# Turned keys and queries with two heads side by side, score products of 64 rows a head, and the low part of x and one mask on other engines

## The chip, the cores and the metric

One core of a Trainium2 chip runs the whole program. The metric is the device time of one execution in microseconds (us), the median of the runs. Engines are named as in the profile: PE is TensorE (matrix products and transposes), PEld its weight loads, DVE VectorE, ACT ScalarE, POOL GpSimd, SP the engine that issues most DMAs.

## The reference

Attention that keeps the 32 largest scores of each row, followed by a gated product, all in float32:

```python
# q, k, v: (4, 8, 576, 64); w_a, w_b: (512, 1536); w_out: (1536, 512)
scores = scale * np.matmul(q, k.transpose(0, 1, 3, 2))
kth = np.partition(scores, -32, axis=-1)[..., -32:-31]
scores = np.where(scores >= kth, scores, -1000000000.0)
scores = scores - np.max(scores, axis=-1, keepdims=True)
attn = np.exp(scores)
attn = attn / (np.sum(attn, axis=-1, keepdims=True) + 1e-09)
x = np.matmul(attn, v).transpose(0, 2, 1, 3).reshape(2304, 512)
out = ((x @ w_a) * (x @ w_b)) @ w_out
```

## The kernel before

**Precision.** A float32 number is split into a high part, which is the number copied to the type fp32r, and a low part, the number minus the high part. Products of fp32r run in one pass over the array. A full product is then three: high by high, high by low, low by high (line 606 for x by w_a and w_b, line 638 for the hidden values by w_out).

**Units and slots.** A unit is 128 queries of a pair of heads (two heads of one batch), or, for the last 64 queries of a batch (the tail), 64 queries of two pairs. There are 72 units: in each of 4 batches 4 blocks of queries by 4 pairs, and 2 tail units. Each engine runs its own program of slots s = 0 to 78, written out by hand, and in slot s it works on different units: DVE finds the 32 largest of unit s, PE makes the scores of unit s+1 (`qk`), turns the probabilities of unit s-1 (`transposes`) and multiplies those of unit s-2 by v (`probs_v`), and the gated product runs 5 slots behind in 72 chunks of 384 columns (chunk n in slot n+5), 4 chunks for each group of 128 tokens. The order inside a slot is fixed; an engine that waits holds up everything behind it.

**PE in slot s:** `probs_v(s-2)`, half of `columns_of(n, 0)` (6 products of 384 columns), `x_subtract(s-2)`, `qk(s+1, 0)`, a part of the keys if one is due (`k_transposes`), the other half of `columns_of(n, 0)`, `qk(s+1, 1)`, `turn_hidden(n-1)`, `transposes(s-1)`, `q_transposes(s+3)`, `output(n-2)` (9 products of 512), `columns_of(n, 1)` (12 products of 384).

**Scores.** A head has 64 rows. The kernel before turns the keys of one head with their high and low part side by side, so that one column of `k_t` holds the high part in rows 0 to 63 and the low part in rows 64 to 127; the query is turned twice over in the same way, and its columns in `q_t` are used with zeros beside them. One product of 128 rows then gives q by (high + low of k); a second, with the low part of q, the rest. Eight products of 288 columns make a unit's scores (16 for a tail unit), in two halves that share the PSUM banks 0 and 1. ACT and POOL split the keys before they are turned (`split_k`, lines 697 and 895), PE turns them in 9 pieces for a pair of heads (line 488), and ACT copies them out (line 709). A pair's keys come in two parts in two slots; there are 12 pairs after the first batch.

**Top 32.** DVE takes the 8 largest four times (line 999) and takes them out in between (line 1016), for both heads of a unit. Then `below` (line 1031) writes `keep` for each head, 0 or -3e38, POOL adds it to the scores (`masked`, line 920), ACT takes the exponential (line 740) and the sum, DVE the inverse (line 1026), and ACT multiplies (line 755). DVE waits for the sums in the middle of the next unit.

**Low part of x.** ACT copies `ps_x` to `x_hi` (line 775), PE subtracts `x_hi` from `ps_x` by a product with the negative identity (line 577), and ACT copies the rest to `x_lo`.

Three score buffers (`ROWS = 3`) let DVE run ahead of PE.

Of the kernel before, what the change touches and what calls it, by code (L numbers as in the profile page):

```python
# [6 lines left out]
def topk_attention_gated_product(nc, q, k, v, w_parts, xs, out):  # L7
    fp32, fp32r = mybir.dt.float32, mybir.dt.float32r
    ALU, ACT = mybir.AluOpType, mybir.ActivationFunctionType

    P = 128
# [16 lines left out]

    PAIR = 2 * S
    TAILS = FULL  # L30

    PARTS_OF_ROW = [(0, FULL * P), (FULL * P, PAIR)]
    KEY_PARTS = [(0, NB * P), (NB * P, PAIR)]
# [47 lines left out]
    NPREPS = 2 * KB * BATCHES  # L81
    PREP_SLOT = [-1] * 4 + [0, 0, 1, 1]
    for b in range(1, BATCHES):
        at = first_unit(b, 0)
        PREP_SLOT += [at + n for n in ((-7, -6, -5, -4, -3, -2, -1, -1) if b % 2 else (-7, -6, -5, -4, -3, -2, -1, 0))]
    for n in range(2 * KB, NPREPS):
        b, p, before = n // 2 // KB, n // 2 % KB, n // 2 - KPAIRS
        assert PREP_SLOT[n] <= first_unit(b, p) - 2
        assert before < 0 or PREP_SLOT[n] >= last_unit(before // KB, before % KB) - 1

# [3 lines left out]
    def split_early(n):  # L94

        return n >= 2 * KB and PREP_SLOT[n - 2] <= PREP_SLOT[n] - 2

    def frees_late(n):

        before = n // 2 - KPAIRS  # L100
        return before >= 0 and PREP_SLOT[n] == last_unit(before // KB, before % KB) - 1

    def parts_until(s):

        return sum(PREP_SLOT[n] <= s for n in range(NPREPS))

# [43 lines left out]
    with ExitStack() as ctx:  # L150
# [13 lines left out]
        neg_ident = sb("neg_ident", [P, P], fp32r)  # L164
        k_rows = [sb("k_rows_a", [P, NB, 2, D]), sb("k_rows_b", [P, FULL, 2, D])]
        q_rows = sb("q_rows", [P, QBUF, 4, 2, D])
        k_t = sb("k_t", [P, KPAIRS, PAIR], fp32r)
        q_t = sb("q_t", [P, 2, 2, 7 * D], fp32r)
        q_whole = sb("q_whole", [P, 2, P])
# [5 lines left out]
        neg_max = sb("neg_max", [P, 2, 2])  # L175
# [3 lines left out]
        probs_t = sb("probs_t", [P, PAIR])  # L179
        x_hi = sb("x_hi", [P, 2, KB, G], fp32r)  # L180
# [6 lines left out]
        leaving = k_t[:, KPAIRS - 1, 0:LOWS * WC].rearrange("p (n c) -> p n c", n=LOWS)  # L187

        ps = ctx.enter_context(nc.psum_tensor("ps", [P, 8, 512], fp32))
        ps_s = ps[:, 0:2, 0:HALF]  # L190
# [6 lines left out]
        ps_q = ps[:, 0:2, HALF:HALF + P]  # L197
# [5 lines left out]
        def keys_in_psum(n):  # L203
            if n < 4:
                return [ps_45, ps_67, ps_67, ps_t][n]
            return ps[:, 6, :] if n == preps_at(PREP_SLOT[n])[0] + 1 else ps_t


        ps_first = [ps[:, 2:4, 0:HALF], ps[:, 4:6, 0:HALF]]
# [3 lines left out]
        def q_columns(u, part):  # L213

            if is_tail(u):
                return q_t[:, u % 2, part, 0:6 * D].rearrange("p (h i c) -> p i h c", h=2, c=D)[:, 0:3:2, :, :]
            return q_t[:, u % 2, part, D:7 * D].rearrange("p (h b c) -> p h b c", h=2, c=D)[:, :, 1:3, :]


        def wo_low(n):  # L220
            if n not in LATE_WO:
                return wo_lo[:]
            at = LATE_WO.index(n) * HB * WC
            return k_t[:].rearrange("p k c -> p (k c)")[:, at:at + HB * WC].rearrange("p (b c) -> p b c", b=HB)
# [13 lines left out]
        def low_of_h(n):  # L238
# [3 lines left out]
            return k_t[:].rearrange("p k c -> p (k c)")[:, at:at + HC]  # L242
# [7 lines left out]
        s_negid = sem("s_negid")  # L250
        ld_k = [sem("ld_ka"), sem("ld_kb")]
# [10 lines left out]
        w_lo_done = sem("w_lo_done")  # L262
        khi_ready = sem("khi_ready")
        klo_ready = sem("klo_ready")
        kt_done = sem("kt_done")
        kt_ready = sem("kt_ready")
# [8 lines left out]
        shift_ready = sem("shift_ready")  # L275
# [11 lines left out]
        xsub_done = sem("xsub_done")  # L287
# [25 lines left out]
        def preps_before(u):  # L313
            b, t, pairs, place = UNITS[u]
            return 2 * (b * KB + max(pairs)) + 2
# [18 lines left out]
        def _(sp):  # L334
            def load_k(n):
                if n >= NPREPS:
                    return
                part = n % 2
                wait(sp, kt_done, n - 1)
                b, p = n // 2 // KB, n // 2 % KB  # L340
                head = b * HEADS + 2 * p
                sp.dma_start(k_rows[part][:, 0:FULL, 1, :],
                             k[head + part, 0:FULL * P, :].rearrange("(t p) d -> p t d", p=P)
                             ).then_inc(ld_k[part], 16)
                if part == 0:
                    for h in range(2):
                        sp.dma_start(k_rows[0][h * TAIL:(h + 1) * TAIL, TAILS, 1, :], k[head + h, FULL * P:S, :]
                                     ).then_inc(ld_k[0], 16)

            def load_q(u):  # L350
# [5 lines left out]
                for twin in range(2):  # L356
                    sp.dma_start(q_rows[0:w, u % QBUF, 0:heads, twin, :],
                                 q[head:head + heads, t * P:t * P + w, :].rearrange("h p d -> p h d")
                                 ).then_inc(ld_q[u % QBUF], 16)

            def load_v(b, p):
# [3 lines left out]
                for h in range(2):  # L365
                    sp.dma_start(v_rows[:, p, 0:FULL, h * D:(h + 1) * D],
                                 v[head + h, 0:FULL * P, :].rearrange("(t p) d -> p t d", p=P)
# [78 lines left out]
            for s in range(FIRST, MOE_END):  # L446
                mine = preps_at(s)
                n = s - MOE0
                for m in range(2, 5):
                    weights(s - 1, m)  # L450
# [630 lines left out]
```

## Time and profile before

| what | us |
|---|---|
| median of 3 runs | 844.06 (843.84 to 845.9) |
| the profiled execution: its time | 845.23 |
| the profiled execution: its span, first to last instruction | 843.4 |
| mean granted TensorE clock | 0.982 of full |

| engine | busy us | share of the span |
|---|---|---|
| PE | 802.1 | 95% |
| PEld | 733.6 | 87% |
| DVE | 772.5 | 92% |
| ACT | 654.2 | 78% |
| POOL | 494.1 | 59% |

Busy time is the union of the instructions' spans; a matmul's span has its latency in it, so a pace is read from starts, or from the chain of work that ended last, which cuts each instruction at the start of the next one.

### The profile page before, as it was taken

What the parts mean: (1) busy time and instruction counts of PE and PEld (TensorE: products, weight loads), DVE (VectorE), ACT (ScalarE), POOL (GpSimd) and SP (SyncE); (2) the same over time, 40 slices, a digit from 0 to 9 for tenths busy, and PEclk for the clock granted to TensorE, in tenths of its full rate; (3) what the DMA queues carried; (4) which work ended last, traced back from release to release, by engine and by line L of the source; (5) the groups of instructions that cost most, each with busy time, mean ns of one, the idle gap of its engine ahead of it and who ended that gap; (6) DMA issues with size and microseconds to landing.
All of it is one profiled execution on the core that took longest, in us unless ns stands there. A gap on an engine that the chain in (4) does not pass through costs nothing.

```text
span 843.4 us, 18267 instructions
## 1 busy us (share of the span) xinstructions
PE 802.1 (95%) x5856; PEld 733.6 (87%) x5856; DVE 772.5 (92%) x1664; ACT 654.2 (78%) x1560; POOL 494.1 (59%) x503
## 2 busy tenths in 40 slices
PE   6458899999999999999999999999999999999998
PEld 4447789989999999999999999998999999999987
DVE  7999999998899999999999999998899999999700
ACT  5888988877778788888877878886777878887632
POOL 3889976655455556566555556665455555555422
PEclk9768999999999999999999999999999999999999
DMA  5576764443554444454644444445363444453562
GB/s 132 151 219 205 228 199 141 118 141 127 153 170 123 146 124 146 124 146 139 166 145 140 130 142 130 135 132 149 110 181 125 141 130 142 126 141 121 149 224 83
DMA packets 136957, 123.88 MB, mean 147 GB/s; under 512 B 81568, under 2 KB 100000, under 8 KB 136864
## 3 DMA queue, kind: packets, MB, share of 16 engines
q1 hardware_dynamic: 136320, 122.58, 49.0%
q8 instruction: 49, 0.80, 0.4%
q14 instruction: 44, 0.36, 0.2%
q10 hardware_dynamic: 544, 0.13, 0.1%
HBM read 113.25 MB, written 9.44 MB: 145 GB/s over the span
## 4 chain that ended last, share of the span: by engine, by line
PE 86%; DVE 7%; SPq 2%; issue 2%; ACT 1%; POOL 1%; DMA 1%; ACTq 0%; POOLq 0%
PE ps L606 35%; PE ps L638 18%; PE ps L566 9%; PE ps L522 9%; PE ps L548 8%; DVE work L1016 3%; PE ps L617 3%; DVE best L999 3%; PE ps L488 2%; PE ps L500 2%; DVE keep L1031 1%; SPq L369 1%; DMA k_rows_a<-in_k 1%; PE ps L577 0%; DMA stage<-in_w 0%
## 5 line engine op out<-in xcount | busy, mean ns | idle before, releaser
L999 DVE MAX8 best<-work 128x8 f32<-128x576 f32 x432 | 305.6, 751 | 0.0
L920 POOL TENSOR_TENSOR scores<-scores,keep 128x576 f32<-128x576 f32 x144 | 218.0, 1534 | 137.1 <-DVE keep L1031 137.1
L1016 DVE MATCH_REPLACE8 work<-best,work 128x576 f32<-128x576 f32 x288 | 213.7, 747 | 0.0
L606 PE MATMUL ps<-w_hi,x_hi 128*128 128x384 f32 x576 | 205.2, 356 | 6.5 <-issue 3.3
L606 PE MATMUL ps<-w_hi,x_lo 128*128 128x384 f32 x576 | 194.7, 338 | 0.0
L927 POOL TENSOR_TENSOR ab<-ab 128x384 f32<-128x384 f32 x72 | 73.3, 1018 | 155.0 <-ACT ab L787 155.0
L606 PE MATMUL ps<-w_lo,x_hi 128*128 128x384 f32 x432 | 146.2, 338 | 0.0
L728 ACT COPY scores<-ps 128x576 f32<-128x576 f32 x142 | 90.8, 640 | 48.6 <-PE ps L522 48.4
L606 PEld LDWEIGHTS ps<-w_hi,x_hi 128*128 128x128 f32 x576 | 108.2, 188 | 22.1 <-issue 15.1
L740 ACT ACTIVATE scores<-scores,neg_max 128x576 f32<-128x576 f32 x144 | 114.2, 808 | 12.6 <-POOL scores L920 12.0
L522 PE MATMUL ps<-k_t,q_t 128*128 128x288 f32 x632 | 116.3, 312 | 4.8 <-ACT scores L728 2.6
L999 DVE MAX8 best<-scores 128x8 f32<-128x576 f32 x144 | 102.3, 753 | 14.0 <-ACT scores L728 11.2
L755 ACT ACTIVATE scores<-scores,inverse 128x576 f32<-128x576 f32 x144 | 112.7, 783 | 2.7 <-DVE inverse L1026 2.4
L606 PEld LDWEIGHTS ps<-w_hi,x_lo 128*128 128x128 f32 x576 | 108.4, 188 | 0.0
L1016 DVE MATCH_REPLACE8 work<-best,scores 128x576 f32<-128x576 f32 x144 | 106.1, 746 | 0.0
L522 PEld LDWEIGHTS ps<-k_t,q_t 128*128 128x128 f32 x632 | 96.7, 197 | 6.9 <-ACT scores L728 4.0
L566 PE MATMUL ps<-probs_t,v_rows 128*64 128x128 f32 (+1 forms) x1600 | 95.1, 267 | 4.2 <-ACT probs_t L765 4.2
L566 PEld LDWEIGHTS ps<-probs_t,v_rows 128*64 128x64 f32 x1600 | 78.5, 137 | 22.4 <-issue 17.0
L638 PE MATMUL ps<-w_hi,h_hi 128*128 128x512 f32 x216 | 91.0, 421 | 0.1
L763 ACT COPY probs_t<-ps 128x512 f32<-128x512 f32 x144 | 81.3, 587 | 10.8 <-PE ps L548 3.4
L548 PE MATMUL ps<-ident,scores 128*128 128x128 f32 x648 | 86.1, 280 | 2.0 <-ACT k_t L709 2.0
L606 PEld LDWEIGHTS ps<-w_lo,x_hi 128*128 128x128 f32 x432 | 81.7, 189 | 3.0
(70 smaller groups left out, 1353.6 us busy)
## 6 DMA issues: line engine op xcount, KB each, us to landing
wo_lo<-x_scratch SPq DMA_DIRECT2D x69, 768.0 KB, 4.5
wb_lo<-x_scratch SPq DMA_DIRECT2D x70, 384.0 KB, 4.1
stage<-in_w SPq DMA_DIRECT2D x36, 256.0 KB, 3.2
q_rows<-in_q SPq DMA_DIRECT2D x142, 64.0 KB, 3.0
x_scratch<-k_t SPq DMA_DIRECT2D x18, 256.0 KB, 2.7
v_rows<-in_v SPq DMA_DIRECT2D x32, 128.0 KB, 2.6
out<-stage SPq DMA_DIRECT2D x16, 256.0 KB, 4.7
k_t<-x_scratch SPq DMA_DIRECT2D x3, 768.0 KB, 6.7
```

The costliest lines, as they stand in the source:

```text
L522: last = mm(ps_s[:, j, :], weights, k_t[:, (b * KB + p) % KPAIRS, at:at + HALF], start=(i == 0), stop=(i == len(terms) - 1))
L548: last = tr(to, row_of(u)[:, at:at + P], ident[:])
L566: last = mm(ps_x[h * D:(h + 1) * D, i * w:(i + 1) * w], v_rows[:, p, block, h * D:(h + 1) * D], probs_t[:, at:at + w], start=(i == 0 and c ...
L606: last = mm(ps_ab[which], x[:, g % 2, kb, :], w, start=(kb == 0 and m == 0), stop=(kb == KB - 1 and m == 2))
L638: last = mm(ps_y, x[:, cols], w, start=(f + b == 0 and m == 0), stop=(f + b == NF - 1 and m == 2))
L728: A.copy(scores[:, u % ROWS, :, half * HALF:(half + 1) * HALF], ps_s[:]).then_inc(s_ready, 1)
L740: A.activation(row, row, ACT.Exp, bias=neg_max[:, u % 2, j:j + 1], scale=SCALE, accum_out=sums[:, u % 2, j:j + 1]).then_inc(e_ready, 1)
L755: A.mul(row, row, inverse[:, u % 2, j:j + 1]).then_inc(p_ready, 1)
L763: A.copy(probs_t[:, a:a + FULL * P], ps[:, 2 + j, :]).then_inc(pt_ready, 1)
L920: V.tensor_tensor(row, row, keep[:, j, :], ALU.add).then_inc(mask_done, 1)
L999: ins = V.max(best[:, u % 2, j, 8 * r:8 * r + 8], src)
L1016: V.match_replace(out=work[:, j, :], in_to_replace=best[:, u % 2, j, 8 * r:8 * r + 8], in_values=src, imm_value=NEG).then_inc(chain, 1)
```

## The change

- `q_transposes` and `k_transposes` turn whole rows with both heads side by side: head 0 in rows 0 to 63, head 1 in rows 64 to 127. Queries take one piece for a unit and not two, keys 5 pieces for a pair of heads and not 9, in one slot. The last piece of the keys has 64 rows.
- The split comes after the turning. ACT copies the turned keys out twice (high part, whole), POOL subtracts; the queries likewise, with 128 columns and not 256.
- `qk` makes three products for each head (high by high, high by low, low by high), each with 64 rows: head 0 in rows 0 to 63, head 1 in rows 64 to 127, in turn. A unit has 12 products of 288 columns (24 for a tail unit), all in one place of the slot, into the banks 0 to 3; `transposes` wait until ACT has copied both halves.
- The subtraction of `x_hi` leaves PE: ACT copies `ps_x` a second time (`x_raw`), and POOL subtracts (`low_of_x`).
- In units 10 to 71 the mask of the second head leaves DVE. ACT computes sign(scale·score - scale·kth) as one byte and writes it over the top byte of `keep`, which holds -3e38: the byte is 0xFF where the score is below, and makes a very small number where it isn't. POOL's `negate` gives it the bias.
- The last blocks of `columns_of(n, 0)` of the first chunk of a group come after `output`.

```diff
-            def qk(u, half):
+            def qk(u):
...
+                wait(pe, klo_ready, pairs_until(u) - 1)
+                wait(pe, k_copied, sum(m <= u - 2 for m in PREP_SLOT[1:]))
+                wait(pe, s_ready, 2 * u)
+                wait(pe, pt_ready, copied(u - 3))
                 for half in range(2):
+                    at = half * HALF
+                    terms = [(0, 0), (0, 1), (1, 0)]
+                    for i, p in enumerate(pairs):
+                        first = i * D if is_tail(u) else 4 * D
+                        for m, (qpart, kpart) in enumerate(terms):
+                            for j in range(2):
+                                rows = slice(j * D, (j + 1) * D)
+                                last = mm(ps_s[half][:, j, :], q_t[rows, u % 2, qpart, first:first + 2 * D],
+                                          k_t[rows, (b * KB + p) % KPAIRS, kpart, at:at + HALF],
+                                          start=(i == 0 and m == 0), stop=(i == len(pairs) - 1 and m == 2))
+                    last.then_inc(qk_done, 1)
...
             def transposes(u, j):
                 pe.wait_ge(p_ready, 2 * u + j + 1)
                 wait(pe, pt_ready, copied(u - 1))
+                wait(pe, s_ready, 2 * min(u + 3, NU))
...
             for s in range(FIRST, MOE_END):
                 probs_v(s - 2)
-                columns_of(n, 0, (0, 1))
-                x_subtract(s - 2)
-                qk(s + 1, 0)
-                for m in preps_at(s)[:1]:
-                    k_transposes(m)
+                columns_of(n, 0, (0,))
+                qk(s + 1)
...
-                columns_of(n, 0, (2, 3))
-                qk(s + 1, 1)
+                columns_of(n, 0, (1, 2, 3)[:3 - len(late_blocks(n))])
...
                 transposes(s - 1, 0)
                 transposes(s - 1, 1)
+                for m in preps_at(s):
+                    k_transposes(m)
                 q_transposes(s + 3)
                 if s < NU:
                     output(n - 2)
+                columns_of(n, 0, late_blocks(n))
                 columns_of(n, 1, (0, 1, 2, 3))
```

ScalarE, in slot s after the two copies of the turned probabilities, and at its end:

```diff
+            def mask_sign(u):
+                if not unit(u) or u < SIGN0:
+                    return
+                act.wait_ge(neg_ready, u + 1)
...
+                act.wait_ge(mask_done, 2 * (u - 1) + 2)
+                A.activation(keep_sign, scores[:, u % ROWS, 1, 0:S], ACT.Sign, bias=neg[:, u % 2, 1, 1:2], scale=SCALE
+                             ).then_inc(keep_ready[1], 1)
...
                 copy_probs_t(s - 1, 0)
                 copy_probs_t(s - 1, 1)
+                mask_sign(s)
                 copy_q(s + 3)
                 weights(s, 3)
                 copy_hidden(n - 1)
-                copy_ab(n, 0)
+                if not late_blocks(n):
+                    copy_ab(n, 0)
+                for m in preps_at(s):
+                    copy_k(m)
```

GpSimd and VectorE:

```diff
+            def negate(u):
...
+                pool.wait_ge(kth_ready, 2 * u + 2)
                 wait(pool, e_ready, 2 * (u - 2) + 2)
+                V.tensor_scalar(neg[:, u % 2, :, :], best[:, u % 2, :, 0:TOPK:TOPK - 1], -SCALE, None, ALU.mult
+                                ).then_inc(neg_ready, 1)
+
+            def low_of_x(u):
...
+                pool.wait_ge(xhi_done, u + 1)
+                pool.wait_ge(xraw_done, u + 1)
+                V.tensor_tensor(low, x_raw[:].rearrange("p (j c) -> p j c", j=len(pairs)), high, ALU.subtract
+                                ).then_inc(xlo_done, 1)
...
                 below(s, 0)
-                below(s, 1)
+                if s < SIGN0:
+                    below(s, 1)
+                elif s == SIGN0:
+                    dve.wait_ge(mask_done, 2 * s)
+                    V.memset(keep[:, 1, :], NEG).then_inc(s_keep, 1)
```

## Rows read from the trace of the kernel before

**Rows 1.** The page: busy us (share of the span) and instructions of an engine.
```profile
PE 802.1 (95%) x5856; PEld 733.6 (87%) x5856; DVE 772.5 (92%) x1664; ACT 654.2 (78%) x1560; POOL 494.1 (59%) x503
```
**Rows 2.** Windows: stretch, length, busy us of each engine, granted clock, DMA share, GB/s.
```profile
20.00:95.00 75.00, 48.45 (x316) 41.81 (x315) 74.04 (x154) 63.24 (x146) 66.67 (x61) 0.80 0.68 194
240.00:340.00 100.00, 100.00 (x778) 92.68 (x778) 100.00 (x219) 80.05 (x192) 56.50 (x58) 1.00 0.46 138
800.00:843.40 43.40, 39.34 (x223) 34.94 (x221) 0.17 (x1) 14.88 (x35) 12.12 (x12) 1.00 0.47 161
```
**Rows 3.** Chain of work, slot s = 39 (start us, us, what).
```profile
442.59 1.24 PE ps L566 x20
...
445.08 0.06 PE ps L577
445.14 0.58 PE ps L522 x4
...
446.77 0.53 PE ps L522 x4
...
447.63 0.98 PE ps L548 x9
448.61 0.22 PE ps L500 x2
...
453.03 1.24 PE ps L566 x20
```
**Rows 4.** Timeline of PE into and out of line 566 (start us, us).
```profile
399.48 0.34 PE L606 MATMUL ps<-w_hi,x_lo 128*128 128x384 f32 x1
399.75 1.31 PE L566 MATMUL ps<-probs_t,v_rows 128*64 128x128 f32 x20
400.99 0.45 PE L606 MATMUL ps<-w_hi,x_hi 128*128 128x384 f32 x1
```
**Rows 5.** Timeline of PE around products of 64 rows, a tail unit's queries.
```profile
187.78 0.60 PE L548 MATMUL ps<-ident,scores 128*128 128x128 f32 x4
188.31 0.46 PE L500 MATMUL ps<-ident,q_rows 64*128 64x64 f32 x4
188.70 0.50 PE L638 MATMUL ps<-w_hi,h_hi 128*128 128x512 f32 x1
```
**Rows 6.** Chain of work: one part of a pair's keys.
```profile
413.93 0.44 PE ps L488 x4
```
**Rows 7.** Timeline of DVE over one unit, from mask to mask.
```profile
405.06 0.93 DVE L1031 TENSOR_SCALAR keep<-scores,best 128x576 f32<-128x576 f32 x2
405.90 1.41 DVE L999 MAX8 best<-scores 128x8 f32<-128x576 f32 x2
...
410.73 0.15 DVE L1026 RECIPROCAL inverse<-sums_eps 128x2 f32<-128x2 f32 x1
...
415.62 0.93 DVE L1031 TENSOR_SCALAR keep<-scores,best 128x576 f32<-128x576 f32 x2
```
**Rows 8.** Timeline of ACT in one slot, [idle before <-releaser].
```profile
433.46 0.27 ACT L775 CAST x_hi<-ps 128x128 fp32r<-128x128 f32 x1 [1.48 <-PE ps L566]
...
436.91 0.64 ACT L728 COPY scores<-ps 128x576 f32<-128x576 f32 x1 [0.26 <-PE ps L522]
...
438.70 0.27 ACT L765 COPY probs_t<-ps 128x128 f32<-128x128 f32 x1
...
441.01 0.81 ACT L740 ACTIVATE scores<-scores,neg_max 128x576 f32<-128x576 f32 x1
...
442.70 0.20 ACT L748 ACTIVATE sums_eps<-sums 128x2 f32<-128x2 f32 x1
```
**Rows 9.** Groups by line: the load of ACT's function table.
```profile
L813 ACT ACT_TABLE_LOAD x1 | 1.3, 1283 | 1.8 <-issue 1.8
```
**Rows 10.** Waits: who waited for whom: us in total, times, longest.
```profile
PE ps L548 <- ACT k_t L709: 2.0, 2, 1.0
```
**Rows 11.** Chain of work at the start: the first unit's scores.
```profile
7.39 2.27 PE ps L533 x8
```

More of the change, by code:

```diff
@@ L241, in low_of_h, with late_blocks @@
             at = len(LATE_WO) * HB * WC + (n - (NCH - 2)) * HC
-            return k_t[:].rearrange("p k c -> p (k c)")[:, at:at + HC]
+            return keys[:, at:at + HC]
+        def late_blocks(n):
+            if not 0 <= n < NCH or n % NH:
+                return ()
+            return (2, 3) if UNITS[PER * (n // NH)][1] == FULL else (3,)
         def row_of(u):
@@ L355, in load_q @@
                 head, w, heads = b * HEADS + 2 * pairs[0], TAIL if t == FULL else P, 2 * len(pairs)
[L356 to L359, printed above, removed]
+                sp.dma_start(q_rows[0:w, u % QBUF, 0:len(pairs), :, :].rearrange("p i h d -> p (i h) d"),
+                             q[head:head + heads, t * P:t * P + w, :].rearrange("h p d -> p h d")
+                             ).then_inc(ld_q[u % QBUF], 16)
             def load_v(b, p):
@@ L477, in k_transposes @@
             def k_transposes(n):
-                part = n % 2
-                pe.wait_ge(klo_ready, n + 1)
-                to = keys_in_psum(n)
-                if n >= 2:
-                    wait(pe, kt_ready, n if to is ps_t else n - 1)
-                if n == 3:
-                    pe.wait_ge(s_ready, 1)
-                if n >= 4 and to is not ps_t:
-                    wait(pe, ab_copied[1], PREP_SLOT[n] - MOE0)
-                for b in range(NB - part):
-                    last = tr(to[:, b * P:(b + 1) * P], k_rows[part][:, b, :, :], ident[:])
+                pe.wait_ge(ld_k[n % 2], 48 * (n // 2 + 1))
+                if n == 2:
+                    pe.wait_ge(klo_first, 1)
+                if n >= KB - 1:
+                    pe.wait_ge(s_ready, 2 * min(PREP_SLOT[n] + 2, NU))
+                for to, a, z in keys_in_psum(n):
+                    for b in range(a // P, -(-z // P)):
+                        w = min(P, S - b * P)
+                        last = tr(to[:, b * P - a:b * P - a + w], k_rows[0:w, n % 2, b, :, :], ident[0:w, 0:w])
                 last.then_inc(kt_done, 1)
@@ L507, in qk @@
                 b, t, pairs, place = UNITS[u]
-                if half == 0:
-                    pe.wait_ge(qt_ready, u + 1)
-                    pe.wait_ge(q_copied, min(u + 2, NU))
-                    wait(pe, kt_ready, preps_before(u))
-                wait(pe, s_ready, 2 * u + half)
-                for j in range(2):
-                    if is_tail(u):
-                        terms = [(q_t[:, u % 2, part, (3 * j + i) * D:(3 * j + i + 2) * D], pairs[i])
-                                 for i in range(2) for part in range(2)]
-                    else:
-                        terms = [(q_t[:, u % 2, part, (2 + 3 * j) * D:(4 + 3 * j) * D], pairs[0])
-                                 for part in range(2)]
-                    at = j * S + half * HALF
-                    for i, (weights, p) in enumerate(terms):
-                        last = mm(ps_s[:, j, :], weights, k_t[:, (b * KB + p) % KPAIRS, at:at + HALF],
-                                  start=(i == 0), stop=(i == len(terms) - 1))
@@ L524, in qk @@
-                last.then_inc(qk_done, 1)
-            def first_scores(j):
-                if j == 0:
-                    pe.wait_ge(qt_ready, 1)
-                pe.wait_ge(kt_ready, j + 1)
-                for half in range(2):
-                    at = j * S + half * HALF
-                    for part in range(2):
-                        last = mm(ps_first[j][:, half, :], q_t[:, 0, part, (2 + 3 * j) * D:(4 + 3 * j) * D],
-                                  k_t[:, 0, at:at + HALF], start=(part == 0), stop=(part == 1))
-                last.then_inc(qk_done, 1)
+                pe.wait_ge(qt_ready, u + 1)
```

288 lines of the change are left out of this document (123 added, 165 removed).

## The prediction

> **What bounds the kernel now.** Four views, in this order. The busy shares name two candidates, PE with 95% and DVE with 92% [rows 1]. The windows tell where each is full: from 20 to 95 us DVE (74.0 of 75 us, clock 0.80, POOL busy 66.7), in the middle both (100.0 of 100 us), and in the last 43 us PE alone, when DVE has ended [rows 2]. Busy shares can't choose between two full engines, so the third view is the chain of work: a whole slot of it is PE and nothing else, from 442.59 to 453.03, 10.44 us [rows 3]. The fourth is DVE's own timeline: from mask to mask 415.62 - 405.06 = 10.56 us without a hole [rows 7]. So DVE needs 10.56 us a unit and PE 10.44 us a slot, but PE has slots with parts of the keys (4 times 0.11 us, [rows 6]) and tail units besides, and it is behind; DVE, up to two units ahead, has that lead to spend. From about 95 us on PE sets the end, and DVE stands 0.1 us behind it: a gain on PE of over 0.1 us a slot is worth nothing for long unless DVE gets faster too. The change cuts both.
>
> **PE, scores of a full unit.** Before: 8 products of 288 columns, 0.58 + 0.53 = 1.11 us, a pace of 0.133 us [rows 3]. After: 12 products of 64 rows. What they cost depends on whether the two heads' products, one in rows 0 to 63 and one in rows 64 to 127, run at the same time. The trace has no such pair. The nearest row is line 566, whose products fill 64 columns of the array each: 20 instructions of 128 columns in 1.24 us [rows 3], where one such float32 pass costs 0.98/9 = 0.109 us when the array is whole (line 548, [rows 3]). Twenty of those would be 2.2 us; they take 1.24, so two run together. That is the split by columns, the change wants the one by rows, and I take it to behave alike: 6 pairs by 0.133 = 0.80 us. Ends: 0.80 us (all together) and 12 by 0.133 = 1.60 us (none).
>
> **PE, changing the shape.** The last full product before line 566 is fed from 399.48 for 0.175 us (the spacing of its neighbours), to 399.66. The first full one after it starts at 400.99 but has 0.45 us and not 0.34, so is fed from 401.10 [rows 4]. Between lie 1.44 us, of which ten pairs by 0.109 are 1.09: going in and out costs 0.35 us. The rows with 64-row products say the same: the last full transpose is fed until 188.22, four small ones at about 0.06 us take 0.24, and the full product after them, 0.50 us long where 0.39 is usual, is fed from 188.81: 0.59 - 0.24 = 0.35 us [rows 5]. `qk` now pays this once a slot: 0.80 + 0.35 = 1.15 us against 1.11. The score products save nothing by themselves.
>
> **A rule against this term.** The weights of each product are loaded separately. The queries' 64-row products follow each other every 0.06 us, each with a load of its own [rows 5]. The Trainium skill (TensorE: Matmul & The Clock Gate, LDWEIGHTS) says that a weight load takes as long for few rows as for 128, since only columns count. By that rule, and if the two loads of a pair don't overlap, each pair would be held by its loads, and the time would be the 873 us of rival C; the row speaks against it.
>
> **PE, the rest of a slot.** The subtraction of x leaves (0.06 us, [rows 3]); what hides its replacement is below. One of two query transposes goes: 0.11 us of 0.22 [rows 3]. Sum for a full unit: +0.04 - 0.06 - 0.11 = -0.13, so 10.31 us. Tail unit: 16 by 0.133 = 2.13 becomes 1.60 + 0.35 = 1.95; the queries lose two pieces of 0.06, the subtraction 0.06: -0.36 us. A pair's keys: 9 by 0.109 = 0.98 becomes 4 by 0.109, one of 64 rows (0.06) and 0.35 for the shape: 0.85, so -0.13. And PE twice waited 1.0 us for the key copies in the middle of a slot [rows 10]; the keys now stand behind `transposes`, and nothing there waits for them before the next slot: -2.0 in all. From 95 us on there are 55 full units, 8 tail units and 12 pairs: 7.2 + 2.9 + 1.6 + 2.0 = 13.7 us less.
>
> **DVE.** Two masks take 0.84 us (405.06 to 405.90, [rows 7]); one leaves from unit 11 on: 10.56 - 0.42 = 10.14 us. That is under PE's 10.31, so all of PE's gain can come out, with 0.17 us to spare. If the mask had stayed, DVE would hold the pace at 10.56.
>
> **ACT.** It idles 1.48 + 0.26 us in front of two waits for PE, and some more between [rows 8]. It gets the sign, 576 elements like the exponential (0.81 us span; with overlap some 0.65), and loses 0.2 us with the narrower queries. The key copies come in one piece, four of about 0.35 us in 12 slots, where they were four in two slots before. So ACT is some 0.45 us fuller a slot and still has room. Two places matter. First, `transposes` now wait for the second half of the scores: x twice, ab, two multiplications and two score copies after `probs_v` end at about 4.5 us into the slot, and PE arrives at 5.0. Second, `mask_sign(s)` waits for DVE's last maximum of unit s, and behind it stand the queries' and hidden values' copies, then the exponentials. That closes a ring: sums of s-1, inverse, rest of DVE's unit (415.62 - 410.73 = 4.89 us, [rows 7]), `negate` with handoffs 0.3, sign 0.65, copies up to the exponential at most 441.01 - 438.70 - 0.16 - 0.2 = 1.95, exponentials 442.70 - 441.01 = 1.69 [rows 8], sums and handoffs 0.3. Together 9.8 us against PE's 10.31: 0.5 us of slack. With key copies 11.2 against PE's 11.16 in such a slot, met by the slack of the next.
>
> **POOL.** It works 0.57 of the time or less in the middle [rows 2]; `low_of_x` (128 columns, under 0.7 us) stands behind `hidden(n-1)`, ready at about 4 us into the slot, and is first read after `output`, at 8. `split_k` moves behind the masks, one piece of about 1.5 us for two of 0.8. Cost nothing.
>
> **A rule for ACT.** The trace holds one load of a function table, 1.28 us [rows 9]. The Trainium skill (ScalarE: Activation LUTs, Table sets) says that functions come in sets and that going to another set costs a load; it doesn't name sign among those that share exp's set. Whether it does, no row shows; if not, the time is that of rival D.
>
> **Start.** The first scores come from 8 products in 2.27 us [rows 11]. The keys are turned without waiting for a split, but the low part is then made from the turned ones and `k_transposes(1)` stands in front of `qk(0)`. Bounds: 1.5 us earlier, 2 later. From 20 to 95 us DVE is full and POOL busy 89% [rows 2]; DVE's own work there is unchanged (the sign begins at unit 10), but POOL gets about 0.4 us a slot, and its masks feed the sums that DVE waits for: 0 to 4 us over 8 slots. I take +2 for both. The last 43 us have no attention work and stay.
>
> **Sum.** 843.4 - 13.7 + 2 = 831.7 us span. The profiled execution takes 1.8 us more than its span, and the median lies 1.2 under it: 832.3, rounded to 832 us.
>
> **Rivals.**
> A, the forecast: pairs run together, PE stays the bound. Its own range is 822 to 840: a pair at 0.12 to 0.145 us and a shape change of 0.25 to 0.45 move 80 unit-equivalents (64 full, 8 double) by up to 8 us. Chance 0.60.
> B, the ring of sign, inverse and sums becomes the bound, at 10.6 us a unit. It decides once sign and handoffs cost over 0.5 us more than assumed. For: ACT was never made to wait for DVE here before, and PE's margin at `transposes` is as small. Price: 0.29 by 61 units = 18 us, 850 us; 841 to 856. Chance 0.14.
> C, slower: the products of the two heads do not run together, in PE's `qk`. Each unit then pays 1.60 + 0.35 and not 1.15, 0.80 by 80 = +64: 896 us. If only their weight loads take turns, at 0.109 us as line 548's: 12 by 0.109 + 0.35 = 1.66, +0.51 by 80 = 873. The two are equally likely. It decides from 0.155 us a pair on, where the gain of 0.13 a slot is gone. For: no row splits by rows. Against: line 566. Chance 0.14.
> D, a table load at each change between sign and exp: 2 by 1.28 in a ring of 9.8 makes 12.4 us a unit, +2.1 by 61 = 128: 960 us. Chance 0.03.
> E, better than A: the shape change for rows costs half, and the freed slack at the start shows: 815 to 822. Chance 0.09.
>
> **How the numbers follow.** 832 is A's time. A, E and nearly all of B lie between 816 and 856, 0.81 together; C and D are left out above. Within 0.3% (2.5 us, what a measurement of this kernel can tell from no change) is 841.5 to 846.6: a piece of B and the seam to A, 0.07. Faster: A, E and a little of B, 0.70. Slower: the rest of B, C and D, 0.23.
>
> **What would show it.** Right: on PE the 12 products start in pairs a few ns apart every 0.13 us, full slots of 10.3 us with no idle, DVE with some 0.2 us of waits a unit, mostly for the inverse. B: ACT waits for `neg` every slot, and PE idles before `transposes` or `probs_v`. C: the 12 products take over 1.3 us. D: many table loads in the groups. Wrong altogether if DVE's early units grow by over 0.5 us.

## The result

| what | us |
|---|---|
| changed kernel, median of 4 runs | 837.09 (836.29 to 837.49) |
| before, median of 4 runs | 844.22 (843.84 to 845.9) |
| ratio, 95% interval | 0.9908 (0.9895 to 0.9922) |
| span of the profiled execution | 835.0, before 843.4 |

It is faster by 0.9%, where 1.4% was forecast; 837.1 lies inside the range and inside case A's own range. The profile of the changed kernel begins with the busy shares, which answer to [rows 1]:

```profile
PE 789.6 (95%) x5960; PEld 685.5 (82%) x5960; DVE 745.8 (89%) x1602; ACT 659.1 (79%) x1614; POOL 507.4 (61%) x560
```

PE has 12.5 us less work, and the span is 8.4 us shorter. The windows, as [rows 2] (stretch, length, busy of PE, PEld, DVE, ACT, POOL, clock, DMA, GB/s):

```profile
20.00:95.00 75.00, 47.47 (x325) 39.49 (x323) 74.52 (x160) 59.96 (x140) 69.59 (x68) 0.93 0.64 183
240.00:340.00 100.00, 98.92 (x756) 86.32 (x755) 96.17 (x208) 82.76 (x205) 59.63 (x67) 1.00 0.39 122
```

In the middle PE is no longer at 100.0 of 100 us. That missing 1.1 us is the first hint. One ordinary slot in the chain of work that ended last, as [rows 3]:

```profile
406.78 1.24 PE ps L555 x20
408.03 0.73 PE ps L586 x3
408.75 1.00 PE ps L521 x11
409.75 1.79 PE ps L586 x9
411.54 0.33 PE ps L597 x3
411.86 0.98 PE ps L537 x9
412.85 0.11 PE ps L497
412.96 2.09 PE ps L618 x9
415.05 2.10 PE ps L586 x12
417.14 1.24 PE ps L555 x20
```

(Line 555 is `probs_v`, 586 `columns_of`, 521 `qk`, 597 `turn_hidden`, 537 `transposes`, 497 the queries, 618 `output`. One of the 12 products of line 521 has no record.) The slot is PE and nothing else: 417.14 - 406.78 = 10.36 us, before 10.44. From `probs_v` to `turn_hidden` it is 4.76 us, before 447.30 - 442.59 = 4.71 us: the score products save nothing, as forecast, and the gain of this slot is mainly the query's single transpose (0.11 and not 0.22 us). The slot that follows has something else in it:

```profile
419.11 0.99 PE ps L521 x12
420.10 1.25 PE ps L586 x6
421.35 0.33 PE ps L597 x3
421.68 0.13 issue
421.80 1.17 PE ps L537 x9
```

Where the 8.4 us lie follows from the starts of `probs_v` of the same units in both traces. The last column divides the terms of the prediction among the stretches:

| from ... to | before | after | difference | forecast |
|---|---|---|---|---|
| start to unit 8 | 124.49 | 123.02 | -1.5 | +2 |
| units 8 to 13 | 54.96 | 55.61 | +0.7 | -1 |
| 13 to 17 (tail units) | 50.05 | 46.42 | -3.6 | -2.7 |
| 17 to 49 | 341.10 | 340.76 | -0.3 | -5 |
| 49 to 53 (tail units) | 50.03 | 46.42 | -3.6 | -2.7 |
| 53 to 71 | 186.62 | 186.76 | +0.1 | -2.3 |
| unit 71 to the end | 36.15 | 36.01 | -0.1 | 0 |

The gain is the tail units and the start. The stretches of full units, on which more than half of the forecast gain stood, brought nothing: +0.7 - 0.3 + 0.1. (The first stretch varies: in experiment 2, whose edit changed nothing, it took 122.47 us, so half a microsecond there says nothing.) So the question for the experiments was: pairs, shape and DVE behave as expected in a slot like the one above, so what takes the gain of the others?

### The profile page after: what moved, and what is told of

The parts are those of the page before. It is cut to its first block, busy times and chain, and to the rows that moved or that the text cites. A ratio compares the mean times of both kernels' runs of the same rounds, so it can differ in the third digit from the quotient of the medians.

```text
span 835.0 us, 18438 instructions
## 1 busy us (share of the span) xinstructions
PE 789.6 (95%) x5960; PEld 685.5 (82%) x5960; DVE 745.8 (89%) x1602; ACT 659.1 (79%) x1614; POOL 507.4 (61%) x560
## 4 chain that ended last, share of the span: by engine, by line
PE 80%; DVE 11%; ACT 3%; issue 3%; POOL 1%; DMA 1%; SPq 0%; ACTq 0%; POOLq 0%
PE ps L586 34%; PE ps L618 17%; PE ps L555 9%; PE ps L537 8%; PE ps L521 7%; DVE work L990 5%; DVE best L973 5%; PE ps L597 2%; DVE keep L1005 1%; ACT scores L737 1%; PE ps L497 1%; PE ps L486 1%; ACT scores L700 1%; DMA x_scratch<-k_t 1%; POOL scores L899 1%
## 5 line engine op out<-in xcount | busy, mean ns | idle before, releaser
L899 POOL TENSOR_TENSOR scores<-scores,keep 128x576 f32<-128x576 f32 x144 | 207.1, 1444 | 28.0 <-ACT keep L713 26.7
L586 PE MATMUL ps<-w_hi,x_hi 128*128 128x384 f32 x576 | 209.9, 364 | 4.6 <-issue 2.3
L745 ACT COPY probs_t<-ps 128x512 f32<-128x512 f32 x144 | 81.7, 588 | 69.6 <-PE ps L537 69.4
L722 ACT ACTIVATE scores<-scores,neg 128x576 f32<-128x576 f32 x144 | 114.5, 823 | 8.8 <-POOL scores L899 8.5
L737 ACT ACTIVATE scores<-scores,inverse 128x576 f32<-128x576 f32 x144 | 114.6, 798 | 1.3 <-DVE inverse L1000 1.2
L555 PE MATMUL ps<-probs_t,v_rows 128*64 128x128 f32 (+1 forms) x1600 | 99.4, 274 | 2.5 <-ACT probs_t L747 2.5
L537 PEld LDWEIGHTS ps<-ident,scores 128*128 128x128 f32 x648 | 75.0, 145 | 31.6 <-issue 19.1
L555 PEld LDWEIGHTS ps<-probs_t,v_rows 128*64 128x64 f32 x1600 | 82.3, 141 | 21.0 <-issue 16.9
L880 POOL TENSOR_SCALAR neg<-best 128x4 f32<-128x4 f32 x72 | 31.1, 433 | 98.6 <-DVE best L973 98.6
L521 PE MATMUL ps<-k_t,q_t 64*128 64x288 f32 x960 | 87.8, 320 | 3.2 <-ACT k_whole L680 1.9
```

What stands on the lines that cost most here:

```text
L521: last = mm(ps_s[half][:, j, :], q_t[rows, u % 2, qpart, first:first + 2 * D], k_t[rows, (b * KB + p) % KPAIRS, kpart, at:at + HALF], star ...
L537: last = tr(to, row_of(u)[:, at:at + P], ident[:])
L555: last = mm(ps_x[h * D:(h + 1) * D, i * w:(i + 1) * w], v_rows[:, p, block, h * D:(h + 1) * D], probs_t[:, at:at + w], start=(i == 0 and c ...
L586: last = mm(ps_ab[which], x[:, g % 2, kb, :], w, start=(kb == 0 and m == 0), stop=(kb == KB - 1 and m == 2))
L722: A.activation(row, row, ACT.Exp, bias=neg[:, u % 2, j, 0:1], scale=SCALE, accum_out=sums[:, u % 2, j:j + 1]).then_inc(e_ready, 1)
L737: A.mul(row, row, inverse[:, u % 2, j:j + 1]).then_inc(p_ready, 1)
```

## The experiments

All medians beside the kernel before on the same chip; ratios with 95% intervals. The times of before on the three chips were 845.74, 845.00 and 844.96 us. The changed kernel's ratio is 0.9908.

**1. The split by rows.** Whole products in place of 64-row ones:

```diff
-                                rows = slice(j * D, (j + 1) * D)
+                                rows = slice(0, P)
```

> The changed kernel where each of the 12 score products of a unit takes all 128 rows and not the 64 of its head. Both heads then get the sum of the two heads' scores: the output is another one, the work of every engine has the same size. What the row split is worth: 12 whole products at 0.133 us are 1.60 us and need no change of shape, against 1.21 us in the trace of the changed kernel; tail units 3.2 against 2.0. Theory: +0.39 by 58 and +1.2 by 8 from 95 us on, +32 us, 866 to 872 us. Rival: whole products cost PE no more, since the pairs of the trace overlap only on paper: 837 us.

Measured 864.31 us, ratio 1.0229 (1.0214 to 1.0244), 27 us over the changed kernel. A slot of its chain:

```profile
420.71 1.58 PE ps L521 x12
422.30 1.58 PE ps L586 x9
```

Twelve products in 1.58 us are one every 0.132 us; with 64 rows they took 0.99 us, and the nine products behind them 1.79 and not 1.58 us. In the trace of the changed kernel the 64-row products start two and two, 3 ns apart, and from the second pair on a pair starts every 0.132 us, so six pairs are 6 × 0.132 us. So going into the shape and out costs (0.99 - 6 × 0.132) + (1.79 - 1.58) = 0.20 + 0.21 = 0.41 us, and the pairs give 0.79 us back. That two heads' products run together is shown, and rival C with it is out. The whole came to 27 us and not to the 29 to 35 expected: an ordinary slot grew by 0.39 us (10.75), but the slots of experiment 4, where PE waits anyway, by 0.13 at most.

**2. The order of the two heads' products.**

```diff
-                        for m, (qpart, kpart) in enumerate(terms):
-                            for j in range(2):
+                        for j in range(2):
+                            for m, (qpart, kpart) in enumerate(terms):
```

> The changed kernel with the 64-row products of a half in another order: three of head 0, then three of head 1, and not in turn. If products of the two heads run together only when they stand next to each other, a half takes 5 or 6 steps of 0.133 us and not 3: +0.53 to +0.80 us a unit, by 80 unit-equivalents +43 to +64 us, 880 to 901 us. Rival: PE lets the second head's products pass into the other half of the rows whatever the order, or they never ran together: no change, 837 us.

Measured 837.12 us, ratio 0.9897 (0.9880 to 0.9913): no change. The chain has the same time for the group:

```profile
418.58 0.99 PE ps L521 x12
```

The theory I had put first is wrong. With three products of head 0 in front of three of head 1, products that start one after the other in program order would need five or six steps of 0.132 us for a half; there are three. The starts say how: the second head's product starts 10 ns behind the first head's, and not 3 ns as when the heads take turns, so the order in the program is seen, but the two heads' rows don't wait for each other.

**3. The price of a shape.** `qk` directly behind `probs_v`, so that PE goes from half columns to half rows without whole products between:

```diff
                 probs_v(s - 2)
-                columns_of(n, 0, (0,))
                 qk(s + 1)
+                columns_of(n, 0, (0,))
```

> The changed kernel with qk(s+1) directly behind probs_v(s-2) on PE, and block 0 of columns_of(n, 0) behind it. A slot then changes from products that fill half the columns straight to products of half the rows, and once back to whole ones: three changes of shape and not four. Theory: each change costs 0.15 to 0.2 us (0.35 us in and out, as the prediction took it), so some 66 slots get 0.15 to 0.2 us shorter, -10 to -13 us, 824 to 827 us, less what PE then waits at the transposes for ACT. Rival: only the way back to whole products costs, or the straight change costs as much as two: no change, 837 us.

Measured 828.24 us, ratio 0.9801 (0.9786 to 0.9815), 8.9 us under the changed kernel. The chain:

```profile
403.09 1.24 PE ps L555 x20
404.33 1.00 PE ps L521 x11
405.33 2.31 PE ps L586 x12
```

1.24 + 1.00 + 2.31 = 4.55 us where the changed kernel has 1.24 + 0.73 + 1.00 + 1.79 = 4.76: one of four changes of shape is saved, 0.21 us a slot. The whole is less than the 10 to 13 us expected, since PE now reaches the transposes earlier and waits there 17 times, 8.0 us in all, where the changed kernel has 8 such waits and 4.1 us; the slots that are first in a group stay at 10.66:

```profile
PE ps L537 <- ACT scores L700: 8.0, 17, 0.9
```

**4. Every fourth slot.** A slot is called here by the unit that it transposes: the slot of unit 24 lies between the starts of `probs_v` of units 23 and 24. In the changed kernel the slot with the first chunk of a group takes 10.66 or 10.67 us, in units 24, 36, 40, 44, 60 and 64 alike; the slot with the "issue" above is one. Its PE timeline (start us, us) shows the hole, and ACT's timeline what PE waits for:

```profile
417.07 1.31 PE L555 MATMUL ps<-probs_t,v_rows 128*64 128x128 f32 x20
...
421.18 0.49 PE L597 MATMUL ps<-ident,ab 128*128 128x128 f32 x3
421.80 1.17 PE L537 MATMUL ps<-ident,scores 128*128 128x128 f32 x9
```

```profile
418.43 0.27 ACT L757 CAST x_hi<-ps 128x128 fp32r<-128x128 f32 x1 [0.75 <-PE ps L555]
418.60 0.27 ACT L760 COPY x_raw<-ps 128x128 f32<-128x128 f32 x1
418.75 0.50 ACT L771 COPY ab<-ps 128x384 f32<-128x384 f32 x1
419.12 0.80 ACT L737 ACTIVATE scores<-scores,inverse 128x576 f32<-128x576 f32 x1
419.81 0.65 ACT L700 COPY scores<-ps 128x576 f32<-128x576 f32 x1
420.32 0.81 ACT L737 ACTIVATE scores<-scores,inverse 128x576 f32<-128x576 f32 x1
421.01 0.65 ACT L700 COPY scores<-ps 128x576 f32<-128x576 f32 x1
```

`turn_hidden` is fed until about 421.51; the second half of the scores is copied at 421.66, and the transposes start at 421.80. ACT's row from 418.43 to 421.66 has no hole: 3.23 us of work behind `probs_v`. PE comes earlier here than elsewhere because in this slot the last block of `columns_of(n, 0)`, three products or 0.53 us, was moved behind `output`. Three kernels take this wait apart. First, the last block back in its place:

```diff
-            return (2, 3) if UNITS[PER * (n // NH)][1] == FULL else (3,)
+            return (2, 3) if UNITS[PER * (n // NH)][1] == FULL else ()
```

> The changed kernel where only groups with tail units do their last blocks of columns_of(n, 0) behind output; all others do blocks 1 to 3 in front of turn_hidden. In the trace of the changed kernel every fourth slot takes 10.67 us and not 10.36, since PE comes 0.5 us earlier to the transposes than ACT's score copies. Theory: these 0.31 us by 15 slots go, -4.6 us, 832.5 us. Rival: PE then waits for the low part of x, which comes from POOL at 3.7 us into the slot where block 3 is reached at about 4.1: no gain, or up to +5 us if the low part is late.

Measured 843.07 us, ratio 0.9969 (0.9958 to 0.9981), 6 us slower than the changed kernel. PE now waits for the low part of x:

```profile
PE ps L586 <- POOL x_lo L891: 10.4, 12, 1.3
```

The edit had a flaw, and the rival (at most +5) came near the size only by luck: `columns_of` waits in front of its first block for the x that its last block needs, so block 1 waited. With the wait in front of block 3 alone:

```diff
-                columns_of(n, 0, (1, 2, 3)[:3 - len(late_blocks(n))])
+                if late_blocks(n):
+                    columns_of(n, 0, (1, 2, 3)[:3 - len(late_blocks(n))])
+                else:
+                    columns_of(n, 0, (1, 2))
+                    columns_of(n, 0, (3,))
```

> As e3_last_block_early, but blocks 1 and 2 of columns_of(n, 0) no longer wait for the low part of x; only block 3 does. In e3_last_block_early PE waited 10.4 us in 12 places for that part, in front of block 1. Theory: block 3 is reached at about 4.05 us into the slot, the low part is there at 3.8, so every fourth slot takes 10.36 us and the time is 832 to 833 us. Rival: the low part comes after 4.05 us, and the slots stay at 10.67: 837 us.

Measured 833.53 us, ratio 0.9865 (0.9849 to 0.9881), and the slots of units 24, 28, 32, 36, 40 and 44 take 10.35 or 10.36 us. Third, the block stays late, but ACT copies the scores first:

```diff
-                normalise(s - 1, 1)
                 copy_scores(s + 1, 1)
+                normalise(s - 1, 1)
```

> The changed kernel with one swap on ACT: the second half of the next unit's scores is copied out in front of the second multiplication by the inverse, and not behind it. Theory: every fourth slot is 0.31 us too long because the transposes wait for this copy, 3.3 us of ACT's work behind probs_v; with the swap it is there 0.65 us earlier and PE no longer waits: -0.31 by 15 and a part of the slots after key copies, -5 to -7 us, 830 to 832 us. Rival: the second multiplication, now last, holds up the second half of the transposes by as much: 837 us.

Measured 832.22 us, ratio 0.9846 (0.9832 to 0.9861), the same slots at 10.34 to 10.38 us. In units 18 to 49 and 54 to 71 together, the kernel before this one takes 3.7 us less than the changed kernel and this one 4.6 us, and in both all of it lies in the slots that are first in a group; the others stay within 0.1 us in sum. Two different edits remove the same 0.31 us; the cause is ACT's row behind `probs_v`, which PE reaches 0.5 us early.

**5. What stands behind the key copies.** POOL's `split_k` behind the low part of x:

```diff
-                for m in preps_at(s - 1):
-                    if m >= KB - 1:
-                        split_k(m)
                 if s < NU + 2 or n >= NCH:
                     hidden_lo(n - 2)
...
                 low_of_x(s - 2)
                 if s >= NU + 2 and n < NCH:
                     hidden_lo(n - 2)
+                for m in preps_at(s - 1):
+                    if m >= KB - 1:
+                        split_k(m)
                 split_q(s + 2)
```

> The changed kernel with POOL's split_k behind low_of_x and hidden_lo, and not in front of them. Theory: the 1.4 us of split_k hold up hidden_lo, this ACT's copy of the second product, and this the transposes on PE in the slot after each of 12 key copies, 0.2 to 0.5 us each: -2 to -5 us, 832 to 835 us. Rival: the longer slots are PE's own work on the keys (0.8 us) and the copies on ACT; then no change, 837 us.

Measured 835.66 us, ratio 0.9879 (0.9864 to 0.9893), 1.4 us less, where 2 to 5 were expected; the span of the profiled execution is 833.2, 1.8 us shorter. The interval of the ratio overlaps with the changed kernel's, so whether it is faster is read from the slots. In the changed kernel the chain of the slot after a key copy goes through POOL:

```profile
156.15 1.39 POOL k_t L864
157.54 0.97 POOL h_lo L915
158.61 0.07 ACT ab L771
```

Slots with a key copy (11.17 us, 0.81 over an ordinary one) stay as they are; the slots after them that are also the first of a group shrink from 10.86 to 10.68 and 10.66 us (units 28 and 32) and from 11.23 to 11.03 (unit 48). By the stretches of the table: 17 to 49 takes 0.75 us less and 8 to 13 0.35 less; the other 0.6 us lie in the start, where they say nothing.

**6. Is DVE's relief needed?** Both masks on DVE, in all units:

```diff
-    SIGN0 = 10
+    SIGN0 = 72
```

> The changed kernel with both masks on DVE in all units (SIGN0 = 72), no sign on ACT. The prediction's step says that DVE then holds the pace at 10.56 us a unit where PE could go at 10.36. Such stretches without keys or tail units are some 34 units long in all: 34 by 0.2 = +7 us at most, less what DVE has as a lead, so 839 to 844 us. Rival: PE's lead over DVE never runs out, and ACT, freed of 0.82 us a unit, comes earlier to the score copies: 833 to 837 us.

Measured 834.93 us, ratio 0.9870 (0.9855 to 0.9885), 2.1 us less than the changed kernel. The forecast step is wrong in its sign. DVE is full again and PE does not wait for it:

```profile
240.00:340.00 100.00, 99.12 (x754) 86.32 (x753) 99.50 (x217) 76.31 (x199) 61.62 (x67) 1.00 0.42 124
```

Where the 2.1 us lie is not where one would look: 1.2 of them in the stretch from unit 8 to 13 (54.43 and not 55.61 us), where the sign begins, and only 0.6 from 17 to 49. In the changed kernel the chain runs there from DVE's last maximum of unit 10, the first with a sign, over `neg` and the sign to the exponentials and back to PE:

```profile
129.03 0.78 DVE best L973
...
129.88 0.42 POOL neg L880
...
130.91 0.04 ACT keep L713
...
134.49 1.52 ACT scores L722 x4
...
140.17 1.17 PE ps L537 x9
```

And the other way round, the sign byte alone on the kernel before (with `negate` in the place of `shifts`, in front of the masks):

```diff
                 below(s, 0)
-                below(s, 1)
+                if s < SIGN0:
+                    below(s, 1)
...
+                mask_sign(s)
                 copy_q(s + 3)
```

> The kernel before with one part of the change alone: the mask of the second head as a sign byte on ACT from unit 10 on, with negate for shifts. DVE's unit falls from 10.56 to 10.13 us, PE's slot stays at 10.43. Theory: PE is the bound in the middle and DVE's relief is worth nothing: within 1.5 us of before. Rival 1: DVE, 0.12 us behind PE, held PE back somewhere: -2 to -5 us. Rival 2: as in the changed kernel, the sign costs ACT's place in the slots with keys and tail units: +1 to +4 us.

Measured 845.58 us, ratio 1.0008 (0.9998 to 1.0017): nothing that is clear of the noise; the largest difference is +0.6 us, again from unit 8 to 13. In neither kernel did taking 0.42 us a unit from DVE bring anything.

**7. The edits together.** `qk` behind `probs_v`, the copy first, `split_k` later:

> The changed kernel with three edits: qk behind probs_v, the copy of the scores first, and POOL's split_k behind the low part of x. If they add up: -11, -6 and -2 us make 818 us. Rival: at a slot of 10.1 us the ring of sign, inverse and sums (9.8 us) or DVE (10.13 us a unit) is reached, and the sum stops at 822 to 828 us.

Measured 819.59 us, ratio 0.9701 (0.9687 to 0.9716). Its slot:

```profile
419.08 1.24 PE ps L555 x20
420.33 0.99 PE ps L521 x12
421.31 2.30 PE ps L586 x12
...
429.23 1.24 PE ps L555 x20
```

429.23 - 419.08 = 10.15 us, and every fourth slot has 10.17 (10.77 where two blocks stand behind `output`). The three gains, 8.9 + 4.9 + 1.4 us, make 15.2; together they are 17.5. The copy first also takes away the waits at the transposes that experiment 3 had paid with: one of 0.4 us is left of 17. At this pace the mask is worth another look:

> e10_together with both masks on DVE in all units. PE's slot is 10.15 us there, so DVE with 10.56 us a unit is 0.41 us slower in stretches without keys and tail units (9 units, then 17 at the end), and its lead over PE, some 5 us to spend, is made good in between. Theory: the lead suffices for all but the last stretch: 0 to +2 us, less 2 us since ACT is freed as in e1_mask_on_dve: 817 to 821 us. Rival: DVE is the bound now and holds most slots at 10.56: 828 to 835 us.

(the last kernel with `SIGN0 = 72`.) Measured 826.42 us, ratio 0.9779 (0.9763 to 0.9795), 6.8 us slower: between the two expectations, and nearer to the rival. The chain between 418 and 450 us has turned over to DVE, and ACT waits for the masked scores:

```profile
by line: DVE work L990 43.8%; DVE best L973 35.7%; issue 14.7%; DVE keep L1005 8.6%; DVE inverse L1000 0.6%
```

```profile
ACT scores L722 <- POOL scores L899: 74.0, 90, 2.1
```

From unit 18 to 26 and from 54 to 62 the slots are as before: there the lead, filled in the tail units, lasts nine units, at 0.41 us each some 3.7 us. After unit 62, and already from 36 on, it is spent: of the nine slots of units 36 to 44 seven take 10.44 to 11.09 us, and only after the key copies of unit 45 they are at 10.15 again. So the lead lasts for a few units, and not for a long stretch. Last, the sign byte from unit 1 on, where DVE is full and PE is not:

```diff
-    SIGN0 = 10
+    SIGN0 = 1
```

> e10_together with the sign byte from unit 1 on and not from unit 10. Up to 95 us DVE is full and PE is not, so here DVE's 0.42 us a unit should come out whole. Theory: -0.42 by 9 units = -3.8 us, 816 us. Rival: in this stretch ACT and POOL split the weights too, and the sums that DVE waits for come later by the sign on ACT: 0 to +4 us, 820 to 824 us.

Measured 816.64 us, ratio 0.9665 (0.9651 to 0.9679), 2.9 us under the one with unit 10, of 3.8 expected. Only half of it is what was expected: the start takes 1.4 us less (120.86 us), and the stretch from unit 8 to 13 1.2 us less (53.08), as little as without any sign (53.11). So the price of the sign in that stretch was that of its beginning at unit 10; whether by the place or because DVE now comes there earlier was not tried. It is the fastest kernel of this study, 20.5 us under the changed one.

## Why the prediction was right in its range and wrong in its size

**What bounds the kernel: right.** PE sets the end from about 95 us on in the kernel before. Experiment 6 confirms it from the other side: DVE's relief alone is worth 0 there. After the change PE still sets it, with ACT's copies for a fraction of a microsecond in every fourth slot.

**PE, scores of a full unit: right.** Pairs at 0.133 us were forecast, 0.132 measured. That the split by rows would behave as line 566's split by columns was assumed and not read; it held.

**Changing the shape: mis-sized.** 0.35 us was read from two places, 0.41 measured (experiment 1). The rows had 64-column weights in one case and four small products in the other; 0.06 by some 66 slots is 4 us, if each slot pays it. The forecast for an ordinary slot was -0.13, measured -0.08. A change of shape costs about 0.2 us each, from half columns to half rows too (experiment 3), so I should have counted changes and not pairs of them. The Trainium skill (TensorEngine Tiling (Array Packing), Key Properties) says that changing the tiling mode drains the array; the trace agrees in that each change costs this 0.21 us, and no row shows what PE does in it.

**A rule against the term.** The rule of the Trainium skill (TensorE: Matmul & The Clock Gate, LDWEIGHTS) on weight loads changed nothing here: two loads of 128 columns start 3 ns apart in the trace of the changed kernel, one for each half of the rows, and a pair of products follows every 0.132 us, the pace of whole products. Whether few rows load faster was not tried; the loads don't hold up the pairs.

**PE, keys and tail units.** A slot with keys was forecast at 11.16 us and is 11.17. The two stretches of tail units brought 7.2 us where 5.4 were forecast, 3.6 and not 2.7 each. The chain of work shows the rest. Before, the first of them (start us, us):

```profile
188.38 0.39 PE ps L500 x4
188.77 2.29 PE ps L638 x9
...
196.82 0.44 PE ps L488 x4
```

After:

```profile
185.56 0.64 PE ps L486 x5
186.20 0.12 PE ps L497 x2
186.32 2.29 PE ps L618 x9
```

Two slots with four small query products save 0.27 us each, and not 0.12 (the other two 0.11); two pairs of keys go from 0.99 to 0.64 us, 0.7 in all and not 0.26, since the small pieces of keys and queries now stand next to each other and pay for one change of shape together, which the queries paid before as well; and the wait for the key copies had cost 1.2 us and not 1.0. These are estimates from the chain, about 0.3 + 0.4 + 0.2 = 0.9 us for each stretch.

**ACT, first place: this step failed.** "About 4.5 us into the slot, and PE arrives at 5.0" was right for an ordinary slot: in experiment 4 ACT's copies end 421.66 - 417.07 = 4.6 us into the slot. But every fourth slot lacks one block of `columns_of(n, 0)` in front, which the diff shows, and there PE arrives at 4.4 (421.51 - 417.07). The step read one slot and applied it to all. Price: 0.31 us a slot, with POOL's part 0.5 in units 28, 32 and 48, and 0.9 in the two slots where two blocks were moved (units 20 and 56: 11.26 us, before 10.55 and 10.57). The two kernels without the 0.31 us are 3.6 and 4.9 us faster, more than the 3.3 us by which the forecast of the span was too low.

**ACT, second place: half right.** The ring of sign, inverse and sums was worked out at 9.8 us and doesn't set the pace in ordinary slots, not even in those of 10.15 us. But the sign takes 0.97 us on ACT and 0.82 until the next start, not 0.65, and twice the ring's chain shows: once where the sign begins, at unit 10 (the rows in experiment 6), and by 0.2 us in each of three slots that follow key copies and are first in a group (the 0.2 us that POOL's edit gives back too). Without the sign the kernel takes 2.1 us less, 1.2 of them at the beginning. Rival B, at 18 us, didn't happen: ACT waited 1.1 us in all for `neg`.

**POOL: mis-sized.** `split_k` cost "nothing" because I counted only its own reader. Behind it in POOL's queue stood `hidden_lo`, behind that ACT's copy of the second product, behind that the multiplications and the score copies: 1.2 us of span behind the start (experiment 5).

**DVE: wrong.** "If the mask had stayed, DVE would hold the pace at 10.56" compared DVE with an ordinary slot. Over units 17 to 49 a slot takes 340.8/32 = 10.65 us on average, keys and first chunks included. That is above 10.56, and three score buffers even it out. From 53 to 71 the average is 186.76/18 = 10.38 us, below 10.56, and still PE took no longer with both masks on DVE (186.75 us, experiment 6): there DVE's lead out of the tail units, whose slots take 12 us, had to pay 18 × 0.18 = 3.3 us, and it did. Experiment 7 shows when the step becomes true: with ordinary slots at 10.15 us, after some 3.7 us of lead.

**Start: wrong in sign.** +2 us forecast, -1.5 measured. POOL did get fuller (69.6 and not 66.7 us from 20 to 95 us), but "DVE's own work there is unchanged" failed. From first maximum to first maximum, DVE's units 1 and 3 took 10.54 us and not 11.76 and 12.18, unit 4 11.95 and not 10.56. The difference is in the masks. One that starts while POOL subtracts the weights (line 886 before, 854 after) can last up to 1.6 us instead of 0.51, until about 0.3 us after the end of that subtraction. Before:

```profile
75.59 1.27 POOL L886 TENSOR_TENSOR k_t<-stage,w_hi 128x512 fp32r<-128x512 f32 x1 [0.25 <-DMA x_scratch<-k_t]
...
75.62 2.00 DVE L1031 TENSOR_SCALAR keep<-scores,best 128x576 f32<-128x576 f32 x2
```

Two masks take 2.00 us there and 0.93 elsewhere [rows 7]. Before the change five masks lasted over 1.1 us, 4.8 us in all above the usual, and after it four, 3.5 us. That is 1.3 us of the 1.5. Which part of the change moved POOL's work so was not tried.

**Table loads:** there is one load in the whole trace, though 62 signs stand among 144 exponentials, so the two share a set, and rival D is out.

**The sum.** The span was forecast at 831.7 us and is 835.0. The other 1.8 of the 5.1 us in the median is that it lies 2.1 us above the profiled span, where 0.6 was taken over from before; the last 0.3 is the rounding to 832. In the span errors cancelled. Against the forecast column of the table, the full units from 17 to 49 and 53 to 71 are 7.1 us short: 4.6 are the waits at the transposes, which the kernel with the copy first gets back there, and the rest is the shape, 50 slots at 0.05 us. Units 8 to 13 are 1.7 us short, 1.2 of them by the sign's beginning. Against this stand -3.5 us for the start and -1.8 for the tail units. So the time lies near the forecast in part by luck: two terms that came out better by 5.3 us hid most of 8.8 us that came out worse.

## What to carry to other kernels

When two engines are near each other, compare their averages over a stretch, keys and odd slots included, and what the buffers between them can lend, not one slot with one unit. When work is moved to another place of a hand-written order, take the slot variants one by one: the waits behind the move show up where a slot lacks the work that used to cover them. Before splitting the array for small products, count the changes of shape and put products of unusual shapes next to each other; here that was worth more than the whole change (8.9 against 7.1 us).

## What was not expected of the hardware

- Products on the two halves of the rows run together even when three of one half stand in front of three of the other in the program: 12 products in 0.99 us in either order (experiment 2). The Trainium skill (TensorE: Matmul & The Clock Gate, The mechanism) says that matmuls start and end in program order; for products on different rows this trace speaks against it: the fourth product of the program starts 10 ns behind the first, and the second 0.24 us behind it.
- Going from half columns straight to half rows costs no more than one change to or from whole products: 4.55 against 4.76 us with one change less (experiment 3).
- A mask of DVE that starts while POOL subtracts weights can take up to 1.6 us and not 0.51; one that starts beside POOL's other work took 0.50 to 0.67 us. This is read from the two traces; no experiment moved POOL's work alone.
- Sign from float32 to every fourth byte takes ACT 968 ns for 576 elements, the exponential 823 ns in the same trace:

```profile
L713 ACT ACTIVATE keep<-scores,neg 128x576 int8<-128x576 f32 x62 | 60.0, 968 | 1.1 <-POOL neg L880 1.1
```
